# Attention matmuls on the whole array instead of in packed pieces, and in other places of the step, in a fused mLSTM and two-MLP kernel

## The reference

```python
# 2 batches, 8 heads, 768 positions, head size 40
for t in range(S):
    m_new = np.maximum(f_gate[:, :, t] + m, i_gate[:, :, t])
    f_stab = np.exp(f_gate[:, :, t] + m - m_new)
    i_stab = np.exp(i_gate[:, :, t] - m_new)
    C = f_stab[..., None, None] * C + i_stab[..., None, None] * outer(vt, kt)
    n = f_stab[..., None] * n + i_stab[..., None] * kt
    y[:, :, t] = sigmoid(o_gate[:, :, t]) * (C @ qt) / np.maximum(np.abs(n @ qt), 1.0)
...
# x: 1536 tokens x 320
xn = x / rms(x) * rms_g
x = (silu(xn @ w_gate) * (xn @ w_val)) @ w_out        # 320 -> 1536 -> 320
h = x @ w_in                                          # 320 -> 2048
return np.maximum(0.01 * h, h) @ w_out2               # 2048 -> 320
```

## Time and profile before

| | us |
|---|---|
| median of 3 runs (lowest, highest) | 469.76 (468.79, 470.19) |
| the profiled execution: its own time | 469.76 |
| the profiled execution: span of the trace | 468.0 |
| up to the first matmul of `gate` | 29.64 |
| steps 0 to 11 of the first MLP | 59.90 |
| steps 12 to 35 (the last with attention beside them) | 132.91 |
| from step 36 to the end | 245.55 |

### The profile page before, as it was taken

How to read it: one execution, slowest core, us unless ns; L and a number is a source line. 1 busy time by engine, 2 the same in 40 slices (tenths; PEclk the granted TensorE clock), 3 DMA queues, 4 the chain that set the end, 5 groups by cost and what they waited for, 6 DMA issues and landing times.

```text
span 468.0 us, 8976 instructions
## 1 busy us (share of the span) xinstructions
PE 430.9 (92%) x3634; PEld 387.2 (83%) x3634; DVE 265.5 (57%) x492; ACT 180.3 (39%) x350; POOL 102.5 (22%) x93
## 2 busy tenths in 40 slices
PE   1658897899999879999999999999999999999997
PEld 1658886889999869899888888888999899989996
DVE  7768768576668687776553333733343433353534
ACT  1563562434324333243433322655334343333332
POOL 1488847303213032100133300442000000000000
PEclk9979899899999999999999999999999999999999
DMA  5867451303123031300021210220000000010101
GB/s 157 291 222 258 169 183 61 117 4 115 55 65 113 5 117 52 115 1 1 29 66 62 62 32 0 63 92 1 0 0 1 2 0 1 0 57 0 57 0 56
DMA packets 21446, 31.41 MB, mean 67 GB/s; under 512 B 1328, under 2 KB 15296, under 8 KB 21408
## 3 DMA queue, kind: packets, MB, share of 16 engines
q1 hardware_dynamic: 21408, 30.87, 20.6%
HBM read 28.85 MB, written 2.02 MB: 66 GB/s over the span
## 4 chain that ended last, share of the span: by engine, by line
PE 68%; DVE 16%; issue 7%; ACT 4%; DMA 2%; POOL 1%; DVEq 0%; SPq 0%; POOLq 0%; ACTq 0%
PE gate_ps L951 20%; PE value_ps L951 19%; PE out_ps L1017 9%; PE out_ps L980 6%; PE even_ps L1017 3%; PE c_ps L1017 3%; PE odd_ps L1017 3%; ACT h_hi L500 2%; PE out_ps L984 2%; DVE hid L754 2%; DVE act_buf L748 2%; DVE state L694 1%; DVE h_lo L767 1%; DMA expo<-decay_scratch 1%; DVE kw L659 1%
## 5 line engine op out<-in xcount | busy, mean ns | idle before, releaser
L767 DVE TENSOR_TENSOR h_lo<-hid,h_hi 128x512 fp32r<-128x512 f32 (+2 forms) x96 | 75.8, 789 | 62.1 <-ACT h_hi L500 62.1
L500 ACT ACTIVATE h_hi<-hid 128x512 fp32r<-128x512 f32 (+2 forms) x96 | 55.5, 579 | 133.4 <-DVE hid L754 95.2
L951 PE MATMUL gate_ps<-x_hi,w_sb 128*128 128x512 f32 (+2 forms) x288 | 70.0, 365 | 15.5 <-DVE act_buf L748 12.7
L951 PE MATMUL value_ps<-x_hi,w_sb 128*128 128x512 f32 (+2 forms) x288 | 70.3, 366 | 0.0
L951 PEld LDWEIGHTS gate_ps<-x_hi,w_sb 128*128 128x128 f32 x288 | 49.0, 190 | 23.7 <-issue 9.2
L951 PEld LDWEIGHTS value_ps<-x_hi,w_sb 128*128 128x128 f32 x288 | 49.6, 192 | 4.8
L980 PE MATMUL out_ps<-h_hi,w_sb 128*128 128x384 f32 (+2 forms) x192 | 49.4, 341 | 0.0
L748 DVE SCALAR_TENSOR_TENSOR act_buf<-act_buf,gate_ps 128x384 f32<-128x384 f32 (+2 forms) x48 | 26.4, 550 | 32.5 <-ACT act_buf L488 32.5
L393 POOL TENSOR_TENSOR w_sb<-raw,w_sb 128x704 fp32r<-128x704 f32 x16 | 27.4, 1716 | 75.7 <-ACT w_sb L482 75.7
L1017 PE MATMUL out_ps<-w_sb,h_hi 128*128 128x320 f32 x192 | 42.8, 308 | 0.0
L951 PE MATMUL value_ps<-x_lo,w_sb 128*128 128x512 f32 (+2 forms) x144 | 40.3, 362 | 0.0
(11 more groups left out here) (168 smaller groups left out, 767.8 us busy)
## 6 DMA issues: line engine op xcount, KB each, us to landing
raw<-in_w SPq DMA_DIRECT2D x12, 544.0 KB, 5.2
expo<-decay_scratch SPq DMA_DIRECT2D x12, 512.0 KB, 5.6
att_sb<-in_tok SPq DMA_DIRECT2D x12, 484.0 KB, 4.7
raw<-in_w SPq DMA_DIRECT2D x16, 352.0 KB, 2.9
att_sb<-in_qk SPq DMA_DIRECT2D x24, 160.0 KB
out_y<-y_acc SPq DMA_DIRECT2D x12, 160.0 KB, 1.9
consts_sb<-in_consts SPq DMA_DIRECT2D x1, 129.5 KB, 3.1
gates_sb<-in_gates SPq DMA_DIRECT2D x1, 96.0 KB, 2.6
```

Of the source, the lines that this page charges most:

```text
L500: nc.scalar.activation(h_hi[:, r, 0:n], hid[:, r, 0:n], ACT.Copy).then_inc(hi_done, 1)
L767: nc.vector.tensor_tensor(h_lo[:, r, 0:n], hid[:, r, 0:n], h_hi[:, r, 0:n].bitcast(F32), ALU.subtract).then_inc(h_done, 1)
L951: last = nc.tensor.matmul(ps[:, 0:n], lhs, rhs, start=(j == 0), stop=(j == len(xs) - 1))
```

## The change

The small attention products are made on the whole array. `from_state` has 4 matmuls (one a pair) with 128 stationary columns and 96 moving ones (`WIDE`) in place of 16; `within` has 8 (one a head) in place of 32; `update_state` has 4 in place of 8, with the weighed keys of both heads of a pair side by side, each padded from 40 to 64 columns. The surplus columns of a result fall on places that the next head writes over or that nobody reads. For this the tiles `kw`, `state` and the value part of `att_sb` are wider (a token row that is loaded grows from 968 to 1024 floats), GpSimd clears `kw` and the stand-in for tile 1 (`weighed(1)`, in `act_buf`), and VectorE handles 64 instead of 40 rows of the state.

The order changes too: TensorE runs `within` in the O round ahead of `gate`, and `update_state` at the end of the R round behind `out1`; VectorE does the second half of the scores product in the R round behind `gated` instead of in the S round ahead of it.

```diff
@@ tensor engine
                 for q in range(PAIRS):
-                    both = slice(q * 2 * DV, (q + 1) * 2 * DV)
-                    for t0 in range(0, P, QP):
-
-                        last = nc.tensor.matmul(inter_ps(n)[t0:t0 + QP, both],
-                                                att_sb[:, n % 2, Q0 + q * P + t0:Q0 + q * P + t0 + QP],
-                                                state[:, n % 2, both], start=True, stop=True)
+                    c0 = q * 2 * DV
+                    last = nc.tensor.matmul(inter_ps(n)[:, c0:c0 + WIDE],
+                                            att_sb[:, n % 2, Q0 + q * P:Q0 + (q + 1) * P],
+                                            state[:, n % 2, c0:c0 + WIDE], start=True, stop=True)
...
-                for h in range(H):
-
-                    rows = slice((h % 2) * HP, (h % 2) * HP + D)
-                    last = nc.tensor.matmul(state_ps(n)[rows, h * DV:(h + 1) * DV], weighed(n)[:, h, :],
-                                            att_sb[:, n % 2, V0 + h * DV:V0 + (h + 1) * DV],
+                for q in range(PAIRS):
+                    c0 = q * 2 * DV
+                    last = nc.tensor.matmul(state_ps(n)[:, c0:c0 + WIDE],
+                                            weighed(n)[:, 2 * q:2 * q + 2, :].rearrange("p z e -> p (z e)"),
+                                            att_sb[:, n % 2, V0 + c0:V0 + c0 + WIDE],
...
                 for h in range(H):
-                    for t0 in range(0, P, QP):
-                        last = nc.tensor.matmul(within_ps(n)[t0:t0 + QP, h * DV:(h + 1) * DV],
-                                                expo[:, n % EXPO, h * P + t0:h * P + t0 + QP],
-                                                att_sb[:, n % 2, V0 + h * DV:V0 + (h + 1) * DV],
-                                                start=True, stop=True)
+                    last = nc.tensor.matmul(within_ps(n)[:, h * DV:h * DV + WIDE],
+                                            expo[:, n % EXPO, h * P:(h + 1) * P],
+                                            att_sb[:, n % 2, V0 + h * DV:V0 + h * DV + WIDE],
+                                            start=True, stop=True)
...
                     for n in work["S"]:
                         scores(n)
+                    for n in work["O"]:
+                        within(n)
...
                     for n in work["R"]:
                         from_state(n)
-                        within(n)
-                        update_state(n)
...
                     out1(s - 1, c, idx)
+                    for n in work["R"]:
+                        update_state(n)
@@ vector engine
                         weigh_keys(n)
                         scores(n, 0)
-                        scores(n, 1)
...
                     for n in work["R"]:
+                        scores(n, 1)
                         from_state(n)
@@ gpsimd
             exponents(0)
 
+            pool.wait_ge(tab_ps, 2)
+            nc.gpsimd.memset(weighed(1), 0.0).then_inc(kw_clear, 1)
             exponents(1)
```

More of the change, by code:

```diff
@@ L56 @@
 HP = 64
-QP = 32
+WIDE = 96
 PAIRS = H // 2
@@ L65 @@
 V0 = 2 * PW
-VW = H * DV
+VW = (H - 1) * DV + WIDE + 1
 KS0 = V0 + VW
@@ L133, in build @@
             expo = sb(first, "expo", [P, EXPO, H * P])
-            kw = sb(first, "kw", [P, H, D])
+            kw = sb(first, "kw", [P, H, HP])
             num = sb(first, "num", [P, 2, H, DV])
@@ L137, in build @@
             xn = sb(first, "xn", [P, DM])
-            state = sb(first, "state", [P, 2, H * DV])
+            state = sb(first, "state", [P, 2, PAIRS * 2 * DV + WIDE])
             c_tab = sb(first, "c_tab", [P, TILES * H])
@@ L144, in build @@
             ms = sb(first, "ms", [P, 2, 4])
-            used = 4 * (2 * ATT + EXPO * H * P + 2 * H * DV + 3 * DM + 2 * H * DV + 4 * TILES * H + 3 * H + 8)
+            used = 4 * (2 * ATT + EXPO * H * P + H * HP + 2 * H * DV + 2 * DM + 2 * (PAIRS * 2 * DV + WIDE)
+                        + 4 * TILES * H + 3 * H + 8)
             if used < 4 * GF * W2:
@@ L180, in weighed @@
         def weighed(n):
-            return act_buf[:, 0, 0:DM].rearrange("p (h e) -> p h e", h=H) if n == 1 else kw[:, :, :]
+            return act_buf[:, 0, 0:H * HP].rearrange("p (h e) -> p h e", h=H) if n == 1 else kw[:, :, :]
         def att_out(n):
@@ L223, in build @@
         p_done = sem("p_done")
+        kw_clear = sem("kw_clear")
         kw_done = sem("kw_done")
@@ L651, in weigh_keys @@
                 dve.wait_ge(tok_in[n % 2], 16 * (n // 2 + 1))
-                if n == 1:
-                    dve.wait_ge(tab_ps, 2)
-                elif n >= FIRST:
+                if n < FIRST:
+                    dve.wait_ge(kw_clear, n + 1)
+                else:
                     dve.wait_ge(dc_done, n)
@@ L658, in weigh_keys @@
                 keys = att_sb[:, n % 2, KS0:KS0 + DM].rearrange("p (h d) -> p h d", h=H)[:, heads, :]
-                nc.vector.tensor_tensor(weighed(n)[:, heads, :], keys, w.broadcast_to(keys.shape), ALU.mult)\
+                nc.vector.tensor_tensor(weighed(n)[:, heads, 0:D], keys, w.broadcast_to(keys.shape), ALU.mult)\
                     .then_inc(kw_done, 1)
@@ L673, in first_state @@
                 for p in range(2):
-                    rows = slice(p * HP, p * HP + D)
-                    st = state[rows, n, :].rearrange("p (q z d) -> p q z d", q=PAIRS, z=2)
+                    rows = slice(p * HP, (p + 1) * HP)
+                    st = state[rows, n, 0:PAIRS * 2 * DV].rearrange("p (q z d) -> p q z d", q=PAIRS, z=2)
                     new = state_ps(n)[rows, 0:PAIRS * 2 * DV].rearrange("p (q z d) -> p q z d", q=PAIRS, z=2)
@@ L686, in update_state @@
                 for p in range(2):
-                    rows = slice(p * HP, p * HP + D)
+                    rows = slice(p * HP, (p + 1) * HP)
                     parts.append((
-                        state[rows, b, :].rearrange("p (q z d) -> p q z d", q=PAIRS, z=2)[:, :, p, :],
+                        state[rows, b, 0:PAIRS * 2 * DV].rearrange("p (q z d) -> p q z d", q=PAIRS, z=2)[:, :, p, :],
                         dec_tab[rows, n * H:(n + 1) * H].rearrange("p (q z) -> p q z", z=2)[:, :, p:p + 1]
-                        .broadcast_to([D, PAIRS, DV]),
+                        .broadcast_to([HP, PAIRS, DV]),
                         c_ps[rows, 0:PAIRS * 2 * DV].rearrange("p (q z d) -> p q z d", q=PAIRS, z=2)[:, :, p, :]))
```

1 line of the change is left out of this document (added).

## The result

| | before | changed |
|---|---|---|
| median, us (lowest, highest; 5 runs each) | 468.79 (467.69, 470.19) | 473.02 (472.62, 473.57) |
| ratio to before, 95% interval | | 1.009 (1.0073 to 1.0108) |
| profiled execution: own time / span, us | 469.76 / 468.0 | 474.08 / 472.3 |
| up to the first `gate` | 29.64 | 31.73 |
| steps 0 to 11 | 59.90 | 59.33 |

The changed kernel is slower by 0.9%, where 465.9 us and "faster" were forecast; 473.0 lies outside the range too. In e6 and e8 those of `within` and the MLP are three higher again.

The account below looks back on a forecast made before the run. TensorE and VectorE were taken to be late in turn in steps 12 to 35, VectorE to carry steps 0 to 11. 469.76 + 0.6 - 0.6 - 0.85 - 3.0 = 465.9 us, range 462.6 to 471.0.

Parts of the forecast that it names:

- distance of a record at full clock: Each whole-array record on TensorE takes 0.083 us, 32 a tile: 2.66 against 1.97 packed, +0.69 us a tile.
- tiles 0 and 1: Ahead of the MLP, longer `within(0)` is covered but `within(1)` delays `finish(1)`: +0.6 us (0 to 1.3).
- steps 0 to 11, order and clock together: Earlier `value` and `gate` give -0.6 us (-1.6 to +2.1); two low-clock stretches vanish, -3.0.
- steps 12 to 35: Seven tiles: TensorE's work +4.8 us, waits of `gate` -6.0, a rest of 0.35 stays: -0.85 (-1.8 to 0.5).
- the opening of a burst: Extra 0.17 us seen at L891, taken off L1034's 0.32 between matmuls, leaving 0.15 to 0.16 a record at half speed.
- The transposes' 0.11: Upper bound for a record: 0.11 us each with 128 columns, if stationary columns set the limit.
- the scaling from packed sets: Four 82-column records side by side in `from_state` take 0.074 us a set; by that rate 96 columns take 0.080.
- The third rival: Loading 128 stationary columns limits a record to 0.108 us, so the kernel gets slower: 474.0 us, chance 0.15.
- the waits: In steps 12 to 35 TensorE's `gate` waits for VectorE six times, 6.0 us in all.
- The order: In steps 12 to 35, `gate`'s waits fall from 6.0 to under 1.5 us, VectorE's for `value` from 12.9 to under 4.
- the tie: In steps 12 to 35, TensorE's 3.3 us behind `value` about match VectorE's chain to `finish`; `finish` waiting for `within` counted as nothing.
- The clock's term: Low-clock stretches behind the 2.52 and 2.79 us waits vanish, saving half of TensorE's busy time: -3.0 us (0 to +3 otherwise).

Follow-up runs that it names:

- e6: The changed kernel with `within` of tiles 0 and 1 alone in packed pieces of 32; 471.39 us.
- e8: The changed kernel with `within` of tiles 2 to 11 in two pieces of 64 positions, 41 moving columns each, in two column groups; 469.35 us.
- e1: The kernel before, its packed pieces kept, with the change's new order on both engines; 464.76 us.
- e5: The kernel before with TensorE's new order alone, VectorE keeping both scores products in the S round; 464.97 us.
- e7: The kernel before with all three packed products behind `out1`, VectorE's `from_state` behind `low`, and the second scores product out of the S round; 461.91 us.
- e3: The changed kernel with 41 moving columns in `within` and 82 in `from_state` and `update_state` in place of 96; 475.65 us.
- e4: The changed kernel with 128 moving columns in place of 96; 473.04 us.
- e2: The changed kernel's whole-array records put back in the order of the kernel before; 487.64 us.
- e9: The changed kernel with 96 moving columns for tiles 0 and 1 alone, 41 and 82 for tiles 2 to 11; 473.48 us.

## Why the prediction was wrong, point by point

The terms, each as forecast and as the profiled executions have it (469.76 + 2.1 - 0.6 + 2.8 = 474.1):

| step of the prediction | forecast | measured |
|---|---|---|
| distance of a record at full clock | 0.083 (0.080 to 0.108) | 0.108 to 0.112 |
| tiles 0 and 1 | +0.6 (0 to 1.3) | +2.1 |
| steps 0 to 11, order and clock together | -0.6 - 3.0 | -0.6 |
| steps 12 to 35 | -0.85 (-1.8 to 0.5) | +2.8 |

**The step that failed first is the price of a record.** It was forecast at 0.083 us and is 0.108, so a tile costs TensorE 1.6 us more and not 0.69. It was read off L1034, the only pair of its kind: 0.32 us from the first to the second at the slow rate, less 0.17 for "the opening of a burst", taken over from L891. That size had no right to stand: L891's products sit in two row groups of 40 rows and came out of a pause, and one pair cannot tell an opening cost from a distance. In the changed kernel, where whole-array records stand ahead of the same pair, its second matmul comes 0.22 behind the first (22.16, and 22.80 - 0.42 = 22.38); in the five traces where packed pieces stand ahead (before, e1, e5, e6, e7) it is 0.32. So some 0.11 was to be taken off, and 0.21 is 0.107 at full clock. The transposes' 0.11 was the better row. The second mistake was the scaling from packed sets: 0.074 for four column groups side by side, 32 stationary columns each, says nothing of 128 columns in one load.

**The third rival is what happened**, with 474.0 for it and 473.02 measured, at a chance of 0.15. Its mechanism is right; that its sum is within 1 us is in part luck. Its terms: steps 12 to 35 +4.4, measured +2.8; tiles 0 and 1 +2.3, measured +2.1; steps 0 to 11 +0.5 less 3.0 for the clock, measured -0.6, so 1.6 too much in one stage stands against 1.9 too little in the other. Both terms of its +4.4 were small: the records cost 11.2 us and not 10.4, and the waits (five in the earlier trace rows, not six) were worth more than the 6.0 that the profile lists. From start to start TensorE's gaps in this stage make 7.3 us more than in a stream, and 132.91 + 11.2 - 135.72 = 8.4 us went in all. The Trainium skill, "TensorE: Matmul & The Clock Gate", section LDWEIGHTS, gives the load of the stationary operand as its columns divided by 1.2, in ns, an estimate of 107 for 128 columns. The trace of the changed kernel agrees at full clock, with 0.108; at the lower rate it shows 0.21, for which that section has no other figure.

**The order did what was forecast.** The waits of `gate` fell from 6.0 to nothing, VectorE's for `value` from 12.9 to 4.9 (forecast under 4), and e1, where the form is left out, gives 464.8. `finish` did come to wait for `within`, in 6 of 7 tiles, one of the prediction's own signs of being wrong: the tie was counted with 0.083 a record.

**The clock's term was mis-sized.** Both low stretches behind steps 4 and 11 are gone, as forecast. But one stands at the head of the MLP now:

```profile
31.80:41.30 9.50, 9.50 (x49) 8.98 (x50) 4.76 (x9) 4.89 (x7) 9.35 (x8) 0.50 0.85 251
```

9.5 us at 0.50, against 3.4 there before and 6.8 behind the two waits, so the mean clock of steps 0 to 11 is 0.92 in place of 0.91. And the price was wrong: half of TensorE's busy time was charged, while VectorE and GpSimd carry the path there. The changed kernel and e3 differ by such a stretch. In the changed kernel the lower rate lasts 9.6 us from the first `gate` on, and the third step's `gate` starts 10.47 us behind the first; in e3 it lasts 4.0 and 8.17. At the end of step 11 2.3 us have become 0.3 (59.33 and 59.02). e4, with 5.5 us, takes 59.09. Where TensorE carries the path, e2's 3.4 us at the lower rate cost some 1.4.

The clock column does not show this for every kernel. In e1 it reads 1.00 up to 39 us, yet the engine works at half speed:

```profile
30.42 1.22 PE L951 MATMUL gate_ps<-x_hi,w_sb 128*128 128x256 f32 x4 [0.96 <-ACT x_odd L468]
...
40.72 0.64 PE L951 MATMUL gate_ps<-x_hi,w_sb 128*128 128x256 f32 x4
```

Four matmuls of `gate` take 1.22 us there, as in e5, whose windows read 0.92 (58.46 us, and 58.71 in e1); the starts of the records give both the same stretch of 9.2 us.

**Tiles 0 and 1** went wrong by the same 0.16 in place of 0.218 at the slow rate: `within(0)` alone was 2.2 us longer and not 1.24, so the 1.69 us by which one of VectorE's operations hung no longer covered it. `finish(1)` starts at 25.37 in place of 22.93, 2.4 later and not 0.6. Of the 2.1 us, 0.66 are not the products': `within(0)` itself starts at 18.67 and not at 18.01, and over all traces that start scatters from 17.5 to 19.8. From it to the first `gate` it takes 12.6 to 13.1 us in the six kernels with whole-array products of 96 or 128 columns there, 11.6 in before and 10.6 to 11.7 in the four others with packed `within`: the hanging operation takes 0.90 to 2.13 us there. e6's medians put the share of `within` at 1.6 us.

## What to carry to other kernels

A stationary side of 128 fp32 columns costs the same whether 41 or 128 columns are streamed against it; a product with few moving columns belongs in pieces of 32 stationary columns side by side. By the packed sets' rate (0.074 us for 82 columns) the two would meet near 120 moving columns, an estimate without the edges of a packed block, and not tried. Where two engines take turns at being late, look at what stands ahead of the instruction that the other waits for: taking two packed products from ahead of `value` was worth 4 us with not one instruction fewer, and putting the whole block behind `out1` 7. Price an operation by rows of its own shape on both sides, and when only one pair exists, keep the far bound as the value until something speaks against it beside an argument.

## What the runs showed of the hardware

- Distance of whole-array fp32 records in these products: 0.108 to 0.112 us at full clock, 0.213 to 0.218 at the lower rate, with 41, 96 or 128 moving columns (the changed kernel, e3, e4). With 64 stationary columns in two column groups 0.066 a pair (e8).
- Each edge between whole-array and packed work costs some 0.10 us: 0.20 a block in before and e7, 0.40 in e1 with its two blocks.
- When the engine first gets faster differs at the start. In the six kernels whose tiles 0 and 1 have 96 or 128 moving columns it does so between 22.3 and 24.6 us, during `within(1)` (2.74 us in the changed kernel, `update_state(0)` 1.06). In e3, with 41 and 82, all products of tiles 0 and 1 stayed at the slow rate (3.53 and 1.98); that went with 2.6 us (e3 against the changed kernel), and e9 gave them back. That the narrow moving side is the cause is not shown: of the four kernels with the same packed start, two got faster at 22 to 23 us (before, e5) and two not before 33.9 (e1, e7).
- A clock of 1.00 in the windows is no proof of full speed at the start: it stood there for the first 20 us in seven traces, and for 39 us of e1, while the matmuls ran at half speed. The records' own distances are the better witness.
